# Thirteen matmuls of the identity in the prologue of an attention and two-MLP kernel on one core

## The reference

```python
scores = scale * np.matmul(q_c, k_full.transpose(0, 1, 3, 2))
scores = scores - np.max(scores, axis=-1, keepdims=True)
a = np.exp(scores)
a = a / (np.sum(a, axis=-1, keepdims=True) + 1e-09)
out[:, :, c_start:c_end] = np.matmul(a, v_full)
```

## Time and profile before

| | before |
|---|---|
| median of 3 timed runs | 1027.58 us (1026.61 to 1027.76) |
| the profiled execution | 1026.84 us, its span 1025.0 us |
| PE busy | 991.7 us (97%), 9792 matmul records |
| PE weight loads | 974.9 us (95%) |
| DVE / ACT / POOL busy | 507.4 / 414.1 / 130.3 us |
| chain that ended last | PE 86%, DVE 5%, DMA 4%, ACT 2% |
| granted PE clock in the 40 slices | 9 tenths or more in each |

### The profile page before, as it was taken

One profiled execution on the slowest core, in us unless ns is written; L12 is line 12 of the kernel. 1 busy time (PEld: TensorE's weight loads), 2 busy tenths in 40 slices (PEclk: granted clock), 3 DMA queues, 4 the chain that ended last, 5 costly groups with the idle time before them and its releaser, 6 DMA issues.

```text
span 1025.0 us, 23197 instructions
## 1 busy us (share of the span) xinstructions
PE 991.7 (97%) x9792; PEld 974.9 (95%) x9792; DVE 507.4 (50%) x1011; ACT 414.1 (40%) x765; POOL 130.3 (13%) x128
## 2 busy tenths in 40 slices
PE   5999999999999999999899999999999999999997
PEld 4999999999999999999899999999999999999997
DVE  4664435243433434342546646565565556555564
ACT  3342222222221212151555555555555555545554
POOL 1123315052320000081100000000000000000000
PEclk9999999999999999999999999999999999999999
DMA  8454455353624320166870202101021110102000
GB/s 359 167 206 138 172 205 197 119 213 125 253 99 166 104 83 2 47 181 208 328 224 21 63 1 61 41 20 41 20 61 27 34 41 20 51 10 61 0 22 21
DMA packets 41798, 108.02 MB, mean 105 GB/s; under 512 B 2816, under 2 KB 29440, under 8 KB 39680
## 3 DMA queue, kind: packets, MB, share of 16 engines
q1 hardware_dynamic: 27904, 79.70, 21.4%
q0 software_dynamic: 13824, 27.27, 8.8%
HBM read 73.40 MB, written 33.55 MB: 104 GB/s over the span
## 4 chain that ended last, share of the span: by engine, by line
PE 86%; DVE 5%; DMA 4%; ACT 2%; issue 1%; POOL 0%; ACTq 0%; DVEq 0%; POOLq 0%
PE mlp L452 23%; PE mlp L454 22%; PE mlp L453 22%; PE attn_ps L445 3%; DMA wc<-wc_scratch 2%; PE scores_ps L421 2%; PE attn_ps L454 2%; PE attn_ps L453 2%; PE attn_ps L452 2%; PE scores_ps L454 2%; PE scores_ps L453 2%; PE scores_ps L452 2%; DMA y_scratch<-y_stage 1%; PE trans_ps L428 1%; PE trans_ps L454 1%
## 5 line engine op out<-in xcount | busy, mean ns | idle before, releaser
L452 PE MATMUL mlp<-y,w_in_hi 128*128 128x256 f32 x768 | 217.8, 284 | 4.5 <-ACT h_copy L602 3.8
L453 PE MATMUL mlp<-y,w_in_lo 128*128 128x256 f32 x768 | 217.3, 283 | 0.0
L454 PE MATMUL mlp<-y,w_in_hi 128*128 128x256 f32 x768 | 217.3, 283 | 0.0
L452 PE MATMUL mlp<-x_hi,w_hi 128*128 128x384 f32 x576 | 197.6, 343 | 3.8 <-issue 2.7
L454 PE MATMUL mlp<-x_lo,w_hi 128*128 128x384 f32 x576 | 193.5, 336 | 0.0
L453 PE MATMUL mlp<-x_hi,w_lo 128*128 128x384 f32 x576 | 193.3, 336 | 0.0
L871 DVE SCALAR_TENSOR_TENSOR g_f<-g_f,h_copy 128x512 f32<-128x512 f32 x96 | 66.4, 692 | 182.2 <-ACT g_f L706 182.2
L452 PEld LDWEIGHTS mlp<-y,w_in_hi 128*128 128x128 f32 x768 | 147.4, 192 | 5.3 <-ACT h_copy L602 4.4
L453 PEld LDWEIGHTS mlp<-y,w_in_lo 128*128 128x128 f32 x768 | 147.4, 192 | 0.0
L454 PEld LDWEIGHTS mlp<-y,w_in_hi 128*128 128x128 f32 x768 | 147.4, 192 | 0.0
L701 ACT ACTIVATE g_f<-mlp,half_col 128x512 f32<-128x512 f32 x96 | 66.0, 688 | 121.2 <-PE mlp L454 121.2
(11 more groups left out here) (97 smaller groups left out, 1991.3 us busy)
## 6 DMA issues: line engine op xcount, KB each, us to landing
qk_raw<-qk_l SPq DMA_DIRECT2D x24, 768.0 KB, 8.1
wc_scratch<-stage_a SPq DMA_DIRECT2D x8, 1792.0 KB, 8.8
wc<-wc_scratch POOLq DMA_DIRECT2D x8, 1792.0 KB, 13.2
v_raw<-v_l SPq DMA_DIRECT2D x24, 512.0 KB, 4.2
y_scratch<-y_stage SPq DMA_DIRECT2D x32, 384.0 KB, 2.5
y<-y_scratch POOLq DMA_DIRECT2D x24, 512.0 KB, 4.9
stage_a<-w SPq DMA_DIRECT2D x6, 768.0 KB, 7.1
stage_b<-w_out SPq DMA_DIRECT2D x8, 512.0 KB, 7.2
```

What stands on the lines that cost most here:

```text
L452: pe.matmul(out_ap, a_hi, b_hi, start=first, stop=False)
L453: pe.matmul(out_ap, a_lo, b_hi, start=False, stop=False)
L454: return pe.matmul(out_ap, a_hi, b_lo, start=False, stop=last)
```

## The change

A helper issues matmuls of `ident` with `ident`, and it is called at five places of the prologue with the counts 4, 2, 1, 2 and 4. The first two write the first 128 columns of `attn_ps`, the other three those of `scores_ps`. Each is a group of its own (`start=True, stop=True`), signals no semaphore, and is overwritten without being read. In front of the third call PE waits until DVE has read the scores of group 2.

```diff
             pe.wait_ge(constants, 1)
             pe.wait_ge(ident_done, 1)
+            def keep_busy(count, bank):
+
+                for _ in range(count):
+                    pe.matmul(bank[:, 0:P], ident[:, :], ident[:, :], start=True, stop=True)
+
             scores_ready(0, 0, 0)
             scores(0)
+            keep_busy(4, attn_ps)
             scores_ready(1, 1, 0)
             scores(1)
+            keep_busy(2, attn_ps)
             transposes(0, 0)
             scores_ready(2, 2, 0)
             scores(2)
             weights_ready(0, 0, 0)
             weighted_v(0)
             transposes(1, 1)
+            pe.wait_ge(sub_done, GPT)
+            keep_busy(1, scores_ps)
             weights_ready(1, 1, 0)
             weighted_v(1)
             transposes(2, 0)
+            keep_busy(2, scores_ps)
             weights_ready(2, 2, 0)
             weighted_v(2)
+            keep_busy(4, scores_ps)
             tile_a(0, 0, True, True)
```

## The result

The kernel after takes 1031.02 us (median of 15 runs, 1028.34 to 1034.23), the kernel before 1027.58 in the same series (15 runs, 1025.64 to 1028.83). The ratio is 1.0037, with a 95% interval of 1.0026 to 1.0047: slower by 0.37%, where 0.4% faster was forecast. The profiled execution took 1030.48 us, its span 1028.7 against 1025.0 before.

What follows compares the result with a forecast made beforehand. PE was taken to bound the kernel, its prologue at the low clock; 2.13 + 1.51 = 3.64 us off 1026.84 gave 1023.20, taken as 1023.5 for the timed runs' offset. Range 1022.5 to 1027.0.

Steps and rivals of the forecast that it cites:

- the levels of the clock read from spacings: Prologue to layer 1: matmul starts 0.32 us apart mean 1.2 GHz, 0.174 mean 2.4 GHz; step between 28.03 and 28.23.
- the fill's price: Prologue: each identity matmul costs 0.45 us at the low clock (0.28 to 0.56), 0.22 at the high (0.30 at most).
- the clock rises early: Prologue, main case: the fill brings the high clock from about 10.5 us on; 3.64 us gained, chance 0.52.
- The trace never shows PE at the high level with light work or short gaps: Argument against the main case: the trace does not say that the high clock holds through the thin prologue stretch.
- the walk from weighted V 0 to weighted V 2: Prologue at high clock, followed along releases and durations: weighted V 2 starts at 19.85, layer 1 at 22.57.
- the term of 2.13 us: Gain in the prologue up to weighted V 2's end: layer 1 starts at 22.57 instead of 24.70.
- the 1.51 in layer 1: First eleven gaps of layer 1 at the high clock: 2.02 us instead of 3.53, 1.51 gained.
- rival 1: Prologue clock rises only in later fills, or falls back between; 2.31 us gained, 1024.5 us; chance 0.16.
- rival 2: Clock rises at about layer 1's start: 1.51 gained less 0.37 delay, 1.14 us, 1025.7 us; chance 0.16.
- a microsecond taken off before the long stream starts at 24.70 comes off the end: PE is busy 64.00 of 64 us from 36 to 100, so prologue gains should shorten the whole kernel.
- rival 4: Fill late at weighted V 2 and layer 1, clock not helped: 1.03 us lost at 0.56 each, 1027.9; chance 0.04.
- the forecast's 3.64 us: Main case's whole gain: 2.13 us in the prologue plus 1.51 in layer 1; chance 0.52.

Runs made afterwards that it cites:

- pad13: Kernel before plus 13 one-column matmuls (52 PE instructions) and the change's wait ahead of layer 1, no fill: 1032.62 us, ratio 1.0070.
- waits52: Kernel before plus 52 PE waits for semaphores reached long ago, in layer 1 of the first tile: 1033.24 us, ratio 1.0064.
- waits52_behind: Kernel before plus 52 PE waits for semaphores reached long ago, in the last tile of phase A, behind the loop: 1024.83 us, ratio 0.9985.
- fill_plus4: Kernel after plus four one-column matmuls (16 PE instructions) behind the last fill: 1024.97 us, ratio 0.9980 to the kernel before.
- wide_fill: Kernel after with the fill's same columns in 5 wide matmuls, 20 PE instructions instead of 52: 1023.11 us, ratio 0.9965 to the kernel before.
- waits_only: Kernel before plus 72 PE waits for semaphores reached long ago, in layer 1 of the first tile, no fill: 1026.29 us, ratio 0.9990.
- waits40: Kernel before plus 40 PE waits for semaphores reached long ago, in layer 1 of the first tile: 1027.87 us, ratio 1.0015.
- wide_waits_late: wide_fill plus 72 idle PE waits in layer 1's first tile, ninth and later loads held until weighted V 0 is done: 1023.62 us, ratio 0.9963.
- pad17: Kernel before plus 17 one-column matmuls (68 PE instructions) in the gap ahead of layer 1, no fill: 1025.99 us, ratio 0.9993.

## Why the prediction was wrong

The forecast was 1023.5 us, and 1031.02 came. The bound, and the levels of the clock read from spacings, were right. So was the fill's price: four identities at the low level start 2.01 us apart from what follows (6.49 to 8.50), 0.50 each, inside 0.28 to 0.56; at the high level four take 1.16 us with their tail, 0.29 each at most; two take 0.71, with the tail in it, against a bound of 0.30 without. That the clock rises early was right, and sooner than priced: within scores 1, not at 10.5 us. Transposes 0 (0.66 for 0.60) and scores 2 (0.85) ran nearly as forecast. One reading was wrong, though it entered the chances only: "The trace never shows PE at the high level with light work or short gaps". The trace before has PE idle for 1.13 and 1.11 us at the jumps, with starts 0.17 to 0.18 apart right behind.

Two steps failed.

The first is the walk from weighted V 0 to weighted V 2 (of weighted V 1: "It takes 1.13 and ends at 18.26"). It counted releases and durations, and took for granted that PE has its instructions. With the break 12 records nearer and PE faster, PE reached the end of its code at 13.48 and stood until 15.16; the clock fell, weighted V 1 took 1.93, weighted V 2 started at 22.15, which is 0.97 late, and took 1.18, and layer 1 started at 24.94. Of the term of 2.13 us nothing came, of the 1.51 in layer 1 all (24.94 to 26.93 is 1.99 for 3.53): with a start 0.24 late, 1.31 net. The clock took the course of rival 1, high at 10 us, low over the middle and high again in weighted V 2; that the size is near rival 2's (1.14) and not rival 1's 2.31 is the stop's doing, which neither had. The sign was in the trace before, in the chain of waits, where weighted V 0 is cut into 25 and 39 records with 0.14 us of "issue" between, and in its 2.38 us against 1.93 for the other two. I took 1.93 and passed over the difference.

The second, which turned the sign, is in the first part: "a microsecond taken off before the long stream starts at 24.70 comes off the end, unless another engine's result becomes late". The 1.31 us did pass on to the jump (1.39 ahead there). But 52 instructions moved the break in the code behind the loop's head from after the 27th pair to after the first, and two jumps cost 3.76 and 3.22 us: 2.4 and 2.0 of stop, and the rest while the granted clock read 0.50. None of the four rivals had this; rival 4, the only one slower than before, put its price at the fill's own place and needed identities of 0.73 us. "Nothing else has moved" held for the order of instructions, not for their addresses, and pad13, waits52 and waits52_behind show that the addresses are what counts.

Without the second fault the forecast of faster would have held: fill_plus4 and wide_fill are 0.20% and 0.35% faster than before. That wide_fill comes near the forecast's 0.4% is in part luck: 0.1% to 0.15% comes without any fill (waits_only, waits52_behind), and its trace shows 0.18 us won in the prologue.

## What to carry to other kernels

Instructions that cost nothing where they stand can cost microseconds at a later jump, as in pad13 and waits52, since they move the loop's head against the pieces in which code is fetched. Before a small edit ahead of a loop is judged, look at the first 3 us behind each jump back for idle time put down to "issue", and time the edit against a control of the same number of idle instructions. If a fill is wanted, choose its number of instructions with that in view: 20 for the same columns were 0.7% faster than 52 here, but 68 (fill_plus4) were 0.6% faster than 52 as well, so it is the place of the break that made most of the difference, not the small number.

## What the runs showed of the hardware

- A stop with "issue" as its cause and no semaphore can be code that has not arrived: at each such stop in the table under Theories a transfer of the instruction queue had ended 1.27 to 1.42 us before PE went on. Behind a jump back it was 1.99 to 2.55 us where one matmul covered it, 1.04 and 1.52 with seven, 0.18 with twelve and five records of scores.
- The clock after such a stop: it fell to 0.50 behind the jumps in the kernel after (2.37 and 2.04 us), stayed at 1.00 in waits40 (1.04 and 1.52), stayed in the prologue of fill_plus4 (1.08) and fell in that of the kernel after (1.68) and of wide_waits_late (1.28). So stops of 1.28 and 1.52 us went either way.
- The break in the prologue came after record 25 of weighted V 0, less the records added ahead of it (13 + 12, 21 + 4), and so after 221 records of PE in every run.
- The 2.4 to 3.0 us until the next piece behind a jump are about 0.2 us until its transfer starts, 0.9 to 1.4 us of transfer and 1.3 to 1.5 us until PE goes on.
- The prologue's stop is 0.14 us in the kernel before and 0.69 in pad13 and pad17, whose code is the same up to there. The transfer starts at 11.98 in the first and at 12.62 and 12.60 in the others.
- Open: why it starts later there; what fills the 1.3 to 1.5 us after a transfer; the second phase's 1.4 to 1.9 us. A kernel whose prologue has no such stop was not found. The most that a trace shows won up to scores 3 is fill_plus4's 2.60 us, so the forecast's 3.64 us stay unshown.
